# Attention, slot experts and feed-forward in fp32: G's first columns by products, a row softmax in two parts, and another order around the experts

## The reference

```python
for t in range(S):                                  # linear attention, per batch and head
    cur = (u * k[t])[:, None] * v[t][None, :]
    y[t] = r[t] @ (state + cur)
    state = w[:, None] * state + k[t][:, None] * v[t][None, :]
x = y as (3072, 384)
logits = x @ phi                                    # (3072, 32)
slot_input = softmax(logits, axis=0).T @ x          # 32 slots, 4 for each of 8 experts
slot_out[e] = relu(slot_input[e] @ w1[e]) @ w2[e]
x = softmax(logits, axis=1) @ slot_out
h = x @ w_in
out = where(h > 0, h, exp(min(h, 0)) - 1) @ w_out
```

## Time and profile before

| | us |
|---|---|
| median of 3 runs | 403.64 (402.93 to 404.47) |
| profiled execution | 403.9 |
| its span in the trace | 402.4 |
| TensorE busy (products) | 389.5, 97% |
| VectorE / ScalarE / GpSimd busy | 267.5 / 220.4 / 103.6 |
| mean granted TensorE clock | 0.987 |

### The profile page before, as it was taken

One profiled execution on the slowest core, in us unless ns is written; L12 is line 12 of the kernel. 1 busy time (PEld: TensorE's weight loads), 2 busy tenths in 40 slices (PEclk: granted clock), 3 DMA queues, 4 the chain that ended last, 5 costly groups with the idle time before them and its releaser, 6 DMA issues.

```text
span 402.4 us, 9718 instructions
## 1 busy us (share of the span) xinstructions
PE 389.5 (97%) x3584; PEld 345.7 (86%) x3584; DVE 267.5 (66%) x510; ACT 220.4 (55%) x505; POOL 103.6 (26%) x129
## 2 busy tenths in 40 slices
PE   7899999999999989998999999999999999999996
PEld 6788888888876444578999999999999999999996
DVE  5667777777764650189987767767767767767771
ACT  2687767676775123195655455554654464455441
POOL 5686767677850000144410000000000000000000
PEclk9699999999999999998999999999999999999999
DMA  7899999999999989930002000200200020002002
GB/s 127 175 256 233 234 230 218 225 235 231 218 319 383 411 329 375 382 95 0 2 0 81 0 2 0 78 0 0 78 0 0 0 78 0 0 0 80 0 2 80
DMA packets 87109, 51.87 MB, mean 129 GB/s; under 512 B 76960, under 2 KB 82208, under 8 KB 85664
## 3 DMA queue, kind: packets, MB, share of 16 engines
q1 hardware_dynamic: 87072, 51.38, 44.8%
HBM read 45.86 MB, written 4.72 MB: 126 GB/s over the span
## 4 chain that ended last, share of the span: by engine, by line
PE 86%; DVE 5%; ACT 3%; issue 3%; DMA 1%; POOL 1%; SPq 0%; DVEq 0%; ACTq 0%; POOLq 0%
PE psum L916 16%; PE psum L917 16%; PE psum L918 16%; PE psum L582 5%; PE psum L827 5%; PE psum L614 5%; PE psum L551 4%; PE psum L622 3%; PE psum L594 3%; PE psum L767 3%; PE psum L605 2%; PE psum L629 2%; ACT scores L1212 1%; DMA u_row<-in_u_dram 1%; PE psum L651 1%
## 5 line engine op out<-in xcount | busy, mean ns | idle before, releaser
L916 PE MATMUL psum<-w_out_hi,elu_hi 128*128 128x384 f32 x372 | 125.3, 337 | 1.4 <-DVE elu_lo L1168 1.4
L917 PE MATMUL psum<-w_out_lo,elu_hi 128*128 128x384 f32 x372 | 125.6, 338 | 0.0
L918 PE MATMUL psum<-w_out_hi,elu_lo 128*128 128x384 f32 x372 | 125.0, 336 | 0.0
L1334 ACT ACTIVATE exp_h<-psum 128x512 f32<-128x512 f32 x95 | 57.1, 601 | 98.6 <-PE psum L827 98.6
L1180 DVE SCALAR_TENSOR_TENSOR elu<-psum,neg_part 128x512 f32<-128x512 f32 x95 | 65.6, 691 | 57.6 <-ACT neg_part L1321 57.6
L917 PEld LDWEIGHTS psum<-w_out_lo,elu_hi 128*128 128x128 f32 x372 | 70.2, 189 | 3.7
L916 PEld LDWEIGHTS psum<-w_out_hi,elu_hi 128*128 128x128 f32 x372 | 70.3, 189 | 1.7 <-DVE elu_lo L1168 1.7
L1168 DVE TENSOR_TENSOR elu_lo<-elu,elu_hi 128x512 fp32r<-128x512 f32 x95 | 70.3, 740 | 0.1
L918 PEld LDWEIGHTS psum<-w_out_hi,elu_lo 128*128 128x128 f32 x372 | 70.3, 189 | 0.0
L1212 ACT ACTIVATE scores<-ident,bonus 128x128 f32<-128x128 f32 x192 | 58.7, 390 | 3.4 <-DVE bonus L959 3.3
L1321 ACT ACTIVATE neg_part<-exp_h 128x512 f32<-128x512 f32 x95 | 59.3, 625 | 0.1
(11 more groups left out here) (168 smaller groups left out, 418.8 us busy)
## 6 DMA issues: line engine op xcount, KB each, us to landing
w_sb<-in_moe_w_dram SPq DMA_DIRECT2D x24, 512.0 KB, 5.0
w<-in_moe_w_dram SPq DMA_DIRECT2D x8, 1536.0 KB, 9.0
r_raw<-in_r_dram SPq DMA_DIRECT2D x24, 192.0 KB, 4.8
k_raw<-in_k_dram SPq DMA_DIRECT2D x24, 192.0 KB, 4.8
v_sb<-in_v_dram SPq DMA_DIRECT2D x24, 192.0 KB, 5.5
out_dram<-out_sb SPq DMA_DIRECT2D x24, 192.0 KB, 1.9
w_in_sb<-in_moe_w_in_dram SPq DMA_DIRECT2D x3, 1024.0 KB, 12.5
w_out_raw<-in_moe_w_out_dram SPq DMA_DIRECT2D x4, 768.0 KB, 11.7
```

The source lines that it names most:

```text
L916: pe.matmul(acc, hi, w_out_hi[:, f, :], start=(f == 0), stop=False)
L917: pe.matmul(acc, hi, w_out_lo[:, f, :], start=False, stop=False)
L918: m = pe.matmul(acc, lo, w_out_hi[:, f, :], start=False, stop=(f == KF2 - 1))
L1334: act.activation(exp_h[:, f % 2, :], banks[4 + f % RING][:, :], ACT.Exp).then_inc(exp_done, 1)
```

## The change

1. **G's first 512 columns** are made by products that write four copies side by side (`G_first`): first columns 0 to 127 in bank 3, then 128 to 511 in bank 2. VectorE casts them to `G_high` and forms `G_T` = G_high x `low_rows` + G, where GpSimd has filled `low_rows` with 0 or -1 for the groups of partitions. `spread`, its products and its copies are gone, and so are the ten warm-up products at L844. The other 1536 columns go to 96 partitions of bank 3 (`G_others`), are split whole by VectorE behind `elu_lo` of f = 0, and moved by the same 12 DMAs, which now start when both parts are there.
2. **The first block f = 0** of the first chunk is done whole, like the others, not in quarters. The order of `ffn_in` in the first four blocks is new, the last batch of f = 0 waits for the split of bank 3, and ScalarE casts w_out for f = 0 and 1 only behind exp and neg_part of f = 0.
3. **w_in** is loaded in two parts by columns (0 to 511, the rest) instead of three by rows.
4. **The row softmax** is done for five chunks (20 units) during the slot products: maximum and subtraction ahead of `logits_T_to_sbuf` of the last chunk, exponential, sum and inverse around `fold_w`, product behind `slot_T`. The last chunk's follows. VectorE no longer waits for D_PARTLO before its relu.
5. **Experts:** half (1,1) comes ahead of the first turn. Both relus come ahead of the copies of `hidden_T`. `turn_weights` has six banks, so that it no longer waits for the copies; three warm-up products instead of four at L811.
6. Tiles of the output layer lie elsewhere in SBUF.

```diff
         w2_sb += [place("w2_7", [P, KF1, DM], F32)]
+        G_high = place("G_high", [P, BANK], F32R)
+        low_rows = place("low_rows", [P, 1], F32)
...
-        cT_banks = (banks[5], banks[6], banks[0], banks[7])
+        cT_banks = (banks[1], banks[2], banks[5], banks[6], banks[0], banks[7])
...
-            for c in range(KD):
-                sp.dma_start(w_in_sb[:, c, :], w_in_dram[:, c, :]).then_inc(w_in_loaded[c], 16)
+            for n, cols in enumerate((slice(0, BANK), slice(BANK, F2))):
+                sp.dma_start(w_in_sb[:, :, cols], w_in_dram[:, :, cols]).then_inc(w_in_loaded[n], 16)
...
-            sp.wait_ge(G_parts_ready, 4)
+            sp.wait_ge(G_parts_ready, 2)
...
+            pool.wait_ge(h_done, NG)
+            pool.memset(low_rows[:, :], 0.0).then_inc(low_rows_set, 1)
+            for n, j in enumerate(range(1, GROUPS, 2)):
+                pool.wait_ge(low_rows_set, n + 1)
+                pool.memset(low_rows[j * GW:(j + 1) * GW, :], -1.0).then_inc(low_rows_set, 1)
...
             expert_in(1, 0)
+            expert_in(1, 1)
             expert_turn(0)
-            expert_in(1, 1)
 
             pe.wait_ge(dve_step, D_PARTLO)
             pe.wait_ge(act_step, A_IDENT_R)
-            pe.wait_ge(hT_ready, 2)
             turn_weights(0)
             turn_weights(1)
             expert_turn(1)
...
-            for _ in range(4):
+            for _ in range(3):
                 pe.matmul(banks[6][:, 0:P], ones[:, :], ones[:, :], start=True, stop=True)
...
+            def G_first(bank, cols, c):
+                for j in range(GROUPS):
+                    m = pe.matmul(bank[j * GW:(j + 1) * GW, cols], slot_out_T[:, c], w_in_sb[:, c, cols],
+                                  start=(c == 0), stop=(c == KD - 1), skip_group_check=True)
+                return m
+
+            def G_others(c):
+                for n in range(1, F2 // BANK):
+                    m = pe.matmul(banks[3][(n - 1) * GW:n * GW, :], slot_out_T[:, c],
+                                  w_in_sb[:, c, n * BANK:(n + 1) * BANK],
+                                  start=(c == 0), stop=(c == KD - 1), skip_group_check=True)
+                return m
...
+            for c in range(KD):
+                m = G_first(banks[3], slice(0, P), c)
+            m.then_inc(G_first_done, 1)
+            G_first(banks[2], slice(P, BANK), 0)
             pe.wait_ge(cT_ready, UNITS // 4)
             pe.wait_ge(G_first_ready, 1)
+            ffn_in(0, 0)
+            G_first(banks[2], slice(P, BANK), 1)
+            G_first(banks[2], slice(P, BANK), 2).then_inc(G_first_done, 1)
+            pe.wait_ge(w_in_loaded[1], 16)
+            G_others(0)
+            G_others(1)
+            pe.wait_ge(G_first_ready, 2)
+            ffn_in(0, 1)
+            G_others(2).then_inc(G_done, 1)
+            for f in range(2, RING):
+                ffn_in(0, f)
...
+                    if first and f < RING:
+
+                        if f == 2:
+                            pe.wait_ge(G_moved[1], 16 * GROUPS)
+                            ffn_in(0, RING)
+                        elif f == 3:
+                            for n in range(RING + 1, 2 * RING):
+                                ffn_in(0, n)
+                    elif f + RING < KF2:
...
+            for n, (bank, cols) in enumerate(((banks[3], slice(0, P)), (banks[2], slice(P, BANK)))):
+                dve.wait_ge(G_first_done, n + 1)
+                dve.tensor_copy(G_high[:, cols], bank[:, cols]).then_inc(G_high_ready, 1)
+                dve.wait_ge(G_high_ready, n + 1)
+                dve.wait_ge(low_rows_set, 3)
+                dve.scalar_tensor_tensor(out=G_T[:, cols], in0=G_high[:, cols].bitcast(F32), scalar=low_rows[:, :],
+                                         in1=bank[:, cols], op0=ALU.mult, op1=ALU.add).then_inc(G_first_ready, 1)
...
+            for f in range(RING):
+                exp_of(0, f, f < 2)
+                neg_of(f, f)
+                if f == 0:
+                    w_out_high(0)
+                if f < RING - 1:
+                    w_out_high(f + 1)
             chunks(act, ffn_group)
```

More of the change, by code:

```diff
@@ L799, in _ @@
             expert_turn(1)
[L800 to L802 removed]
+            pe.wait_ge(hT_low_ready, 1)
+            pe.wait_ge(hT_high_ready, 1)
+            turn_weights(2)
+            turn_weights(3)
+            turn_weights(4)
+            turn_weights(5)
+            pe.wait_ge(cT_ready, 1)
             expert_out(0, range(KF1))
[L804 removed]
+            pe.wait_ge(cT_ready, 2)
+            pe.wait_ge(hT_low_ready, 2)
+            pe.wait_ge(hT_high_ready, 2)
             expert_out(1, range(KF1 // 2))
@@ L827, in ffn_in @@
                 pe.matmul(banks[4 + f % RING][:, :], G_T[:, f * P:(f + 1) * P],
                           c_T[:, bass.ds(i * BANK, BANK)], start=True, stop=True).then_inc(ffn_done, 1)
-            def ffn_in_first(b):
-                pe.matmul(banks[4 + b][:, 0:P], G_T[:, 0:P], c_T[:, b * P:(b + 1) * P],
-                          start=True, stop=True).then_inc(h_first, 1)
-            def spread_G(bank, cols):
-                for part in range(2):
-                    m = pe.matmul(bank, spread[0:GW, part], G_parts[0:GW, part, cols],
-                                  start=(part == 0), stop=(part == 1))
-                m.then_inc(G_spread, 1)
@@ L842, in keep_clock_up_in @@
-            def keep_clock_up_in(bank, n):
-                for _ in range(n):
-                    pe.matmul(bank[:, 0:P], ones[:, :], ones[:, :], start=True, stop=True)
-            pe.wait_ge(spread_ready, 3)
-            keep_clock_up_in(banks[2], 6)
-            pe.wait_ge(G_parts_ready, 2)
-            spread_G(banks[0][:, 0:P], slice(0, P))
+            pe.wait_ge(soT_ready, 2)
+            pe.wait_ge(w_in_loaded[0], 16)
+            for c in range(KD):
+                m = G_first(banks[3], slice(0, P), c)
@@ L866, in first_out_low @@
-            def first_out_low(b):
-                pe.wait_ge(lo_first, b + 1)
-                return pe.matmul(banks[b][:, 0:DM], elu_lo[:, 0, b * P:(b + 1) * P], w_out_hi[:, 0, :],
-                                 start=False, stop=False)
-            pe.wait_ge(w_out_ready, 1)
-            first_out_high(0)
-            pe.wait_ge(G_rest_ready, 1)
-            for b in range(1, B):
-                pe.wait_ge(elu_first, b + 1)
-                ffn_in(0, b)
-                first_out_high(b)
-                first_out_low(b - 1)
@@ L1151, in first_lo @@
-            def first_lo(b):
-                dve.wait_ge(hi_first, b + 1)
-                return dve.tensor_tensor(elu_lo[:, 0, quarter(b)], elu[:, 0, quarter(b)],
-                                         elu_hi[:, 0, quarter(b)].bitcast(F32), ALU.subtract).then_inc(lo_first, 1)
-            first_elu(0)
-            first_hi(0)
-            dve.wait_ge(G_spread, 2)
-            dve.tensor_copy(G_T[:, P:BANK], banks[1][:, 0:BANK - P]).then_inc(G_rest_ready, 1)
-            for b in range(1, B):
-                first_elu(b)
-                first_lo(b - 1)
-                first_hi(b)
@@ L1182, in ffn_group @@
                                              ).then_inc(elu_done, 1)
-                    if not (first and f <= 2):
+                    if not first:
                         elu_lo_of(i, (f - 1) % KF2, q - 1)
-                    dve.wait_ge(elu_done, q)
+                    dve.wait_ge(elu_done, q + 1)
                     if f >= RING:
```

233 lines of the change are left out of this document (95 added, 138 removed).

## The result

| | us |
|---|---|
| changed kernel, median of 19 runs (18 without the one of 756.18) | 400.94 (400.91) |
| kernel before, median of 19 runs beside them | 403.92 |
| ratio | 0.9938 (95% interval 0.9918 to 0.9957) |
| profiled execution, its span | 402.08, 400.3 |

What follows compares the result with a forecast made beforehand. TensorE's products bound the output loop, so only reaching f = 4 earlier helps: 1.2 + 0.25 + 3.5 gave 4.95 us; 403.64 - 5.0 = 398.6 us, own range 397.6 to 399.6, 8-in-10 range 396.6 to 401.0.

Steps and rivals of the forecast that it cites:

- The diff leaves its repeating part alone.: Output loop: its repeating part is unchanged, so the program ends earlier only if that state is reached earlier.
- Experts, 1.2 us: Experts: the fourth block ahead of the first turn removes 1.22 us of TensorE idle; gain 1.2 us, bounds 0.9 to 1.3.
- everything keeps its length: Experts, behind the relu: lengths stay unchanged, so the second products start at 151.05 instead of 152.26 us.
- Rival (a): Output layer's start: the clock falls once in the new, shorter waits, costing 1.7 us, to 400.3; chance 24%.
- The relu hidden by two weight turns: Experts, second group: two weight turns (0.89 us) cover its relu and hand-overs (0.8 us), with nothing to spare.
- Row softmax, 0: End of attention: softmax in two parts fits into idle time and gains 0 us (-0.1 to 0.2).
- w2_7, 0 to 1.1: Experts' weight DMA: landing at 155.0 costs nothing, at 157.4 costs 1.1 us; 0 was taken.
- One warm-up product fewer, 0.25: Ahead of the last turn: one warm-up product fewer gains 0.25 us (0 to 0.27).
- Start of the output layer, 3.5: From G's first products to f = 4: the new start-up gains 3.5 us, 1.7 of it the slow clock not returning.
- the wait for bank 3: f = 0, last batch: TensorE waits 0.8 us for VectorE to empty bank 3 (0.2 if the cast is not held).
- wait for elu_hi of f = 1: Output layer's start, behind f = 0: TensorE waits another 0.1 to 0.8 us for VectorE's cast.
- the move of G: Ahead of f = 2: TensorE waits 0.4 us (0 to 1.1) for G's next columns, moved by SP.

Runs made afterwards that it cites:

- l1_tiles: Kernel before with only the SBUF places of exp_h, elu_hi, elu and elu_lo changed to the changed kernel's; 405.54 us against 403.78, ratio 1.0047.
- o1_experts: Kernel before with only the new experts order, both relus ahead of the copies and six banks for turned weights; 403.32 us against 403.78, ratio 0.9978.
- m1_whole_softmax: Changed kernel with the row softmax whole and behind slot_T again, the new experts order kept; 400.90 us.
- c1_elu: Kernel before with only elu moved to the low region; 2.320 us per block, 401.43 us in one run.
- l3_shift: Kernel before with G_parts, neg_part, w_in_sb, exp_h, elu, elu_hi and elu_lo 32 bytes higher; 2.326 us per block, 404.93 us in one run.
- w1_warm: Changed kernel with elu_lo some 9 KB higher and two warm-up products on each of two waits ahead of the experts; 398.90 us, ratio 0.9852.
- c3_after_lo: Changed kernel with elu_lo some 9 KB higher, starting at the same place as elu_hi modulo 8 KB; 399.83 us, ratio 0.9889.
- s2_start_only: Changed kernel with the old experts order and the whole row softmax behind slot_T; 402.15 us against 404.82, ratio 0.9934.
- l2_elu_lo: Kernel before with elu and elu_lo at the changed kernel's places, elu_hi 4 KB lower; 2.340 us per block, 405.56 us in one run.

## Where the prediction failed and where it held

- **"The diff leaves its repeating part alone."** This step failed. I read the loop's instructions and not the addresses of its tiles; item 6 of the change was costed at nothing, without a reason. It takes 1.84 us in the profile, 1.9 in l1_tiles: about three quarters of the 2.5 us that are missing from the gain by the ratio. None of the rivals had it.
- **Experts, 1.2 us.** The mechanism is right (no idle ahead of the turn; 1.4 us from first product to second layer in o1_experts). What failed is "everything keeps its length": in the profiled execution the clock falls at 136 and the products take 1.5 us more, and by their mean clock six more of the 18 had such a fall. As an estimate, 1.5 us in 7 of 18 is 0.6 on average; with the 1.84 of the tiles this is 2.4 of the 2.5 that are missing. Rival (a) had the price nearly right (1.7 for 1.5) and the place wrong: it looked for the fall in the new waits, not in an old wait (0.50 and 0.45 us ahead of the experts) behind which the cover had been taken away. I had named that 1.22 us of idle only as a loss; it was also what absorbed a slow clock.
- **The relu hidden by two weight turns.** TensorE waits 0.21 us for it ([0.21 <-DVE hidden] above): the two turns do not quite cover it, as "nothing to spare" had left open.
- **Row softmax, 0.** Right, and m1_whole_softmax says the same of what it buys. Its first two steps ended at 128.39 and the copy behind them began at 128.51, the inverses ended 0.41 us ahead of den_cols.
- **w2_7, 0 to 1.1.** 0 in the profiled execution, 1.1 in one of m1_whole_softmax.
- **One warm-up product fewer, 0.25.** From the second layer to G's first product 12.63 us instead of 165.12 - 152.26 = 12.86: 0.23.
- **Start of the output layer, 3.5.** Measured 21.72 - 17.89 = 3.8 from G's first product to the first product with w_out of f = 4. Against kernels of the old start in which the clock didn't fall at 183 (o1_experts, l1_tiles, c1_elu, l3_shift: 20.31 to 20.33) it is 2.4; so the fall cost 1.4, where the sum had 1.7. In all nine profiles with the new start the clock is at 1.00 from 140 to 188: rival (a) did not come. That the total fits is partly luck, since terms inside are off both ways: first w_out product 7.29 us behind G's first (6.6 worked out), since VectorE's first cast began 0.93 us behind G's first product (0.8 worked out from the row; the lower estimate of 0.6 would have been further off), the multiply-adds took 0.35 and 0.61 and each hand-over some more; the wait for bank 3 hardly there (0.1 instead of 0.8), as TensorE came later; no wait for elu_hi of f = 1 (0.1 to 0.8); the move of G 0.52 us late (0.4).
- **Sum.** Without a fall the changed kernel takes 399.93 to 400.94, and once 403.60. 398.6 + 1.8 for the tiles is 400.4. With elu_lo placed well and no fall, w1_warm takes 398.90 and c3_after_lo 398.36 and 399.07: near the 398.6 that had been forecast for the change as it was meant, though the kernel before had its usual falls in the 403.64 from which that was worked out.

## What to carry to other kernels

When a change moves tiles, read the pace of one period of the loop from the trace before and after: here 0.9% in the loop took back half of what the start-up gave. If the pace has changed with the same instructions, try the weights' tile at another offset modulo 256 bytes, and first at the one that it had. An idle stretch behind a place where the clock may fall is a cover; whoever removes it should fill the waits ahead of it, here with four warm-up products. And times that fall in groups are read by their granted clock before medians are compared.

## What was not expected of the hardware

- A block of 13 products (twelve with 384 streamed columns, one with 512) took 2.320 us when elu_hi, elu_lo, w_out_hi and w_out_lo stood at one place modulo 256 bytes, and was up to 1.1% slower when weights did not: 2.334 and 2.340 us with elu_lo 64 and 128 bytes off, 2.326 and 2.346 with elu_hi and elu_lo both 32 and 128 off. The granted clock was 1.00 in all, from 250 to 284 us. Which part of the path this comes from, and against which of the other tiles the distance counts, no run shows.
- The granted clock fell to 1.2 GHz for some 3.4 us at 136 us in some executions and not in others, behind two waits of 0.45 and 0.50 us. TensorE had been busy 1.64 of the 2.50 us from 134 on in s2_start_only, where it fell, and in c3_after_lo, where it did not. With 2.44 of 2.50 it did not fall in the two profiles, and by the mean clock in none of the ten executions.
- w2_7, a DMA of 1.57 MB, took 6.9 us (l2_elu_lo) to 10.6 us (m1_whole_softmax) to land.
